# State rows in one transfer per half, and the division of a on VectorE: an attention and two MoE layers on one core

## The reference, cut to what matters

```
B, H, S, Ns, D = 8, 8, 512, 32, 64
scores = scale * x @ state^T          # [B, H, S, Ns]
a  = exp(scores - max);  a  /= a.sum(-1)  + 1e-9       # "a": rows over the states
xread = a @ state
scores2 = scale * state @ x^T         # the same products, transposed
a2 = exp(scores2 - max); a2 /= a2.sum(-1) + 1e-9
sread = a2 @ x
x = concat([xread, sread], rows)      # 8 batches of 512 + 32 rows, 512 columns
x = ((x @ w1) * (x @ w2)) @ w3 @ w_out            # moe1, d_ff 1024
h = x @ w_in;  out = (h - tanh(h)) @ w_out2       # moe2, d_ff 2048
```

## Time and profile before

| | |
|---|---|
| time, median of 3 runs | 1258.31 us (1258.15 to 1258.31) |
| the profiled execution's own time | 1258.3 us |
| its span | 1256.2 us |
| busy: TensorE, VectorE, ScalarE, GpSimd | 1245.0, 792.2, 546.5, 16.0 us |
| granted clock of TensorE | 1.00 up to 1254 us |
| front stage | 0 to about 112 us; ys to 121, moe1 to about 513 us |
| transfers | 63.75 MB, nearly all in the first 66 us at above 400 GB/s |

### The profile page before, as it was taken

How to read it: one execution, slowest core, us unless ns; L and a number is a source line. 1 busy time by engine, 2 the same in 40 slices (tenths; PEclk the granted TensorE clock), 3 DMA queues, 4 the chain that set the end, 5 groups by cost and what they waited for, 6 DMA issues and landing times. The chain is left out here.

```text
span 1256.2 us, 17133 instructions
## 1 busy us (share of the span) xinstructions
PE 1245.0 (99%) x6652; PEld 1003.6 (80%) x6652; DVE 792.2 (63%) x1282; ACT 546.5 (44%) x1023; POOL 16.0 (1%) x14
## 2 busy tenths in 40 slices
PE   8999999999999999999999999999999999999998
PEld 6779777777777778888888888888888888888887
DVE  4656555545454434788667676676676676776766
ACT  5663333333333333545444344344444444444443
POOL 0000000000000000000000000000000000000000
PEclk9999999999999999999999999999999999999999
DMA  9930100000000112211100101001001001010000
GB/s 373 401 115 27 59 34 1 34 35 1 34 34 1 52 53 81 84 51 51 51 10 14 44 18 51 1 17 50 0 17 50 8 9 50 17 42 0 8 34 17
DMA packets 18109, 63.75 MB, mean 51 GB/s; under 512 B 1920, under 2 KB 3200, under 8 KB 14080
## 3 DMA queue, kind: packets, MB, share of 16 engines
q1 hardware_dynamic: 17712, 62.59, 13.6%
q10 hardware_dynamic: 336, 0.33, 0.1%
HBM read 45.09 MB, written 17.83 MB: 50 GB/s over the span
## 5 line engine op out<-in xcount | busy, mean ns | idle before, releaser
L1208 ACT ACTIVATE hq<-bank 128x512 f32<-128x512 f32 (+1 forms) x144 | 82.8, 575 | 395.7 <-PE bank L1334 395.7
L1279 DVE TENSOR_TENSOR hw<-hw,hq 128x512 f32<-128x512 f32 (+1 forms) x144 | 95.5, 663 | 194.9 <-ACT hw L1219 194.7
L1334 PE MATMUL bank<-ysp_hi,wi_hi 128*128 128x512 f32 (+1 forms) x576 | 217.3, 377 | 0.0
L1334 PE MATMUL bank<-ysp_lo,wi_hi 128*128 128x512 f32 (+1 forms) x576 | 217.3, 377 | 0.0
L1334 PE MATMUL bank<-ysp_hi,wi_lo 128*128 128x512 f32 (+1 forms) x576 | 217.3, 377 | 0.0
L1360 PE MATMUL wide<-wz_hi,gsp_hi 128*128 128x512 f32 x544 | 212.5, 391 | 1.4 <-DVE gsp_lo L1269 1.3
L1360 PE MATMUL wide<-wz_lo,gsp_hi 128*128 128x512 f32 x544 | 211.8, 389 | 0.0
L1360 PE MATMUL wide<-wz_hi,gsp_lo 128*128 128x512 f32 x544 | 211.8, 389 | 0.0
L1334 PEld LDWEIGHTS bank<-ysp_hi,wi_hi 128*128 128x128 f32 x576 | 108.4, 188 | 20.6
L1334 PEld LDWEIGHTS bank<-ysp_lo,wi_hi 128*128 128x128 f32 x576 | 108.2, 188 | 20.4
L1334 PEld LDWEIGHTS bank<-ysp_hi,wi_lo 128*128 128x128 f32 x576 | 108.3, 188 | 20.0
(11 more groups left out here) (127 smaller groups left out, 1748.5 us busy)
## 6 DMA issues: line engine op xcount, KB each, us to landing
y_dram<-ysb SPq DMA_DIRECT2D x8, 1024.0 KB, 4.3
out<-ysb SPq DMA_DIRECT2D x8, 1024.0 KB, 4.6
yr<-y_dram SPq DMA_DIRECT2D x28, 256.0 KB, 4.1
xs<-in_x_rows SPq DMA_DIRECT2D x6, 1024.0 KB, 9.0
xT<-in_x_cols SPq DMA_DIRECT2D x5, 1024.0 KB, 10.6
w_raw<-in_moe_w SPq DMA_DIRECT2D x8, 512.0 KB, 8.3
wi_raw<-in_moe_w_in SPq DMA_DIRECT2D x4, 1024.0 KB, 7.1
raw<-in_moe_w_out SPq DMA_DIRECT2D x16, 256.0 KB, 2.6
```

The lines of the kernel that those rows point to most:

```text
L1208: act.activation(hq[:, f % 2, 0:w], ph[f % 2][:, 0:w], ACT.Square).then_inc(sq_done, 1)
L1279: dve.tensor_tensor(u, u, q, ALU.mult).then_inc(w2_done, 1)
L1334: mm = pe.matmul(ph[f % 2][:, 0:w], wi[s][c][:, f * P:(f + 1) * P], ysp[k][u][c][:, 0:w], start=c + m == 0, stop=c == KC - 1 and m == LAST)
```

## The change

Four edits:

- The state rows of a half are stored by one transfer (four batches) in place of four.
- The division of `a` by its sums is done by VectorE, directly before the transpose back, in place of GpSimd. In the front stage batch 0's division and transpose back stand behind `split_w3(6)`.
- In the rounds of the front stage VectorE does `split_sr` and `split_w3` ahead of batch 0's sum and reciprocal (e = 4) and of its division and transpose (e = 5).
- SyncE issues the load of w3's slice 2 ahead of x by columns of batch 2, and slice 5 and x of batch 5 ahead of x of batch 6.

```diff
-    def gpsimd_scale(self, pool, e):
-        pool.wait_ge(self.row_inv, e + 1)
+    def vector_scale(self, dve, e):
+        dve.wait_ge(self.row_inv, e + 1)
         a = self.room(e)
-        pool.tensor_tensor(a, a, self.rinv[:, :].unsqueeze(2).to_broadcast([P, J * H, NS]), ALU.mult).then_inc(self.scaled, 1)
+        dve.tensor_tensor(a, a, self.rinv[:, :].unsqueeze(2).to_broadcast([P, J * H, NS]), ALU.mult).then_inc(self.scaled, 1)
...
         for e in range(2, 5):
+            if e == 2:
+                load_w3(sp, e)
             load_xT(sp, e)
-            load_w3(sp, e)
+            if e > 2:
+                load_w3(sp, e)
             for n in ((0,), (1, 2), (3,))[e - 2]:
                 load_w(sp, n)
             load_xs(sp, e)
-        load_xT(sp, 6)
         load_w3(sp, 5)
         load_xT(sp, 5)
+        load_xT(sp, 6)
...
-        for e in range(B):
-            rows.gpsimd_scale(pool, e)
...
+            split_sr(e - 1)
+            if e < NF1 - 1:
+                split_w3(e + 1)
             if e == 4:
                 rows.vector_sum(dve, 0)
                 rows.vector_invert(dve, 0)
             if e == 5:
+                rows.vector_scale(dve, 0)
                 rows.vector_back(dve, 0)
-            split_sr(e - 1)
-            if e < NF1 - 1:
-                split_w3(e + 1)
             empty_prod(e)
...
         rows.vector_invert(dve, 1)
+        rows.vector_scale(dve, 1)
         rows.vector_back(dve, 1)
...
                     if f == 7:
+                        rows.vector_scale(dve, b + 2)
                         rows.vector_back(dve, b + 2)
...
     def store_states(eng, j):
-        for n in range(P // NS):
-            eng.dma_start(out_v[j * (P // NS) + n, S:ROWS, :], ob[n * NS:(n + 1) * NS, j, :]).then_inc(o_out, 16)
+        batches = slice(j * (P // NS), (j + 1) * (P // NS))
+        eng.dma_start(out_v[batches, S:ROWS, :], ob[:, j, :]).then_inc(o_out, 16)
...
-        sp.wait_ge(o_out, 16 * 2 * B)
+        sp.wait_ge(o_out, 16 * (B + 2))
```

## The result

The changed kernel takes 1263.25 us (median of six runs, 1263.21 to 1265.79) against 1258.41 us for the kernel before on the same chip (six runs, 1258.15 to 1258.56): a ratio of 1.0042 (that of the medians is 1.0038), 95% interval 1.003 to 1.0054. By the medians it is slower by 4.8 us, where 4.3 had been forecast. The sixth took 1265.79.

What follows compares the result with a forecast made beforehand. The prediction took TensorE, busy 1245.0 of 1256.2 us, to bound the kernel, followed by a tail of stores. 1258.3 + 0.2 (front) + 4.1 (tail) = 1262.6 us; range 1260.0 to 1265.0.

Steps and rivals of the forecast that it cites:

- Tail: Final state-row stores: each merged transfer uses the same four DMA engines, 64 rows each at 0.10 us; +4.1 us.
- 16 engines: Rival for the final stores: all 16 engines take each merged transfer; −0.6 us there, 1257.9 us in all; chance 0.13.
- different engines for the two halves: Rival for the final stores: four engines each, but not the same four; +1.6 us, 1260.1 in all; chance 0.06.
- The fixed 1.56: Final stores: the fixed us per transfer, 1.8 − 2 × 0.12, to which the time of the rows is added.
- the shorter issues: Final stores: SyncE's and ScalarE's issue, 0.4 in place of 1.8 us, gains nothing because the engines end last.
- The landings of 5 to 9 us: Sign in the changed profile's final stores: transfers landing that late would show the forecast right, near 2.5 us wrong.
- Front: Front stage: gains at batches 2 and 5 against a loss at batch 6, −0.25 − 0.75 + 1.2 = +0.2 us.
- Iteration 5: Front stage, batch 5: the 1.26 us wait for w3's low part goes, exponentials come later; gain 0.65 to 0.8 us.
- Iteration 6: Front stage, batch 6: division and transpose back on VectorE delay tokens_max(6) and the exponentials; loss 1.1 to 1.3 us.
- The loads at batch 2: Front stage: w3 lands some 2.5 us sooner, x at about 28.0; gain 0.20, up to 0.28 us.
- The exchange of x 5 and x 6: Front-stage loads: brings x 5 forward; no wait for either is in the trace, so it gives nothing.
- The other seven divisions: ys and moe1 stages: moving them to VectorE costs nothing; if cover is gone, 0.1 us twice.

Runs made afterwards that it cites:

- store_only: The kernel before with only the merged stores, one transfer per half: 1263.29 us, ratio 1.0037.
- store_pairs: The kernel before with two batches per store transfer, two transfers per half: 1268.77 us, ratio 1.0084.
- store_serial: The kernel before with merged stores, ScalarE issuing its half only when SyncE's has landed: 1266.59 us, ratio 1.0064.
- front_x6_back: The changed kernel with stores in four transfers per half and x of batch 6 loaded ahead again: 1258.40 us, ratio 1.0003.
- low_ahead_w3: The kernel before with w3's low part ahead of batch 0's sum and w3's slice 2 loaded ahead of x of batch 2; division on GpSimd: 1257.77 us.
- front_only: The changed kernel with the stores in four transfers per half as before: 1258.57 us, ratio 1.0001.
- gap_division: front_x6_back with batch 0's division and transpose back at the head of round 5, where VectorE is idle: 1257.27 us, ratio 0.999.

## Why the forecast came out right, point by point

**Tail, +4.1 forecast, +4.8 measured.** The mechanism held: four engines, the same for both halves, 64 rows each, 256 packets of 2 KB and 8 small ones, a share near 0.25, 9.1 us from the first issue to the end. The rivals of 16 engines and of different engines for the two halves fall by the share of 0.26 in the changed kernel, and again by `store_only` and `store_pairs`. But that +4.1 is so near +4.8 is in part luck: two errors offset each other. A row costs 2048 B / (102 / 4 GB/s) = 0.080 us, the lower bound, and not the 0.10 that I took; 64 rows are 5.1 and not 6.4 us, −1.3. Against that stands a term that I didn't have: 1.56 + 5.1 + 0.4 makes 7.1, and it was 9.1, so the slow begin costs 2.0 us. In `store_serial` the same sum for one half gives 1.95 (6.07 − 1.56 − 32 × 0.080). The fixed 1.56, worked out from transfers on 16 engines, was thus the mis-sized term: for these it is about 3.5 (1.56 + 1.95 to 2.0). The remark on the shorter issues (nothing gained) was right. That the chain would end in a transfer was wrong: it ends in VectorE's `ysb`, as before, since it doesn't follow the last stores. The landings of 5 to 9 us can't be read, as the profile gives none for these transfers.

**Front, +0.2 forecast, between 0.0 and +0.1 measured** (+4.84 us for the change and +4.77 for the stores alone, +0.05 for the rest, each against the kernel before on its chip). Its steps:

*Iteration 5.* As forecast: the wait of 1.26 goes, a wait of 0.33 for the exponentials takes its place (0.4 expected), `tokens_max(5)` at 58.46 (58.57 expected). The gain is 0.9 us from 62.31 to 61.41, of which 0.06 was there already at the transposes of batch 4 (52.16 against 52.22); 0.75 had been expected.

*Iteration 6.* The division costs 1.17 us in `front_x6_back`, within 1.1 to 1.3. In the changed kernel it lies under the wait for x, so the TensorE wait of 1.2 us foretold for its trace is not there; there VectorE's `tokens_max(6)` comes at 68.78 and waits 0.34.

*The loads at batch 2.* x landed 8.4 us after its issue at 19.58, at 28.0 as forecast, and w3's slice 6.3 us after 19.20, at 25.5. The scores of batch 2 start at 29.33 without a wait on a transfer, and the 0.20 is gone from the trace. ScalarE's wait for the slice, 0.53 in the earlier trace rows, is gone as well. But the forecast took for fixed a wait of TensorE that varies: four of seven traces with the old order lack it (see `low_ahead_w3`), so its absence here does not credit the exchange, and the times show too little to tell the gain from nothing. One figure ahead of the prediction is off: of the 63.75 MB some 25 MB, not nearly all, move in the first 66 us (343 GB/s up to 18 us, 399 from there to 66).

*The exchange of x 5 and x 6 "gives nothing".* This is the step that failed. I looked only for a wait that the exchange could remove, and didn't ask what the queue has to do while the load now in front waits for its buffer. From 46 to 50 us it moves 217 GB/s in the changed kernel's trace, where it moved 402, and 315 in the next two, where it moved 420; the rows of x for batch 5 land 9.8 us after their issue (8.0 before), and TensorE waits 1.60 us for them. The sum survived it because that wait and the division's stall cover each other: in the traces the changed kernel loses 1.72 us there and `front_x6_back` 1.17, not the sum of two losses. The 0.55 between them is as much as this execution lies above its kernel's median, so in a usual execution the exchange may cost nothing at all; in the medians it stays unresolved. What a long wait can cost besides is in the trace of `front_only`, with the fall of the granted clock.

*The other seven divisions.* Nothing, as forecast: TensorE's wait for `pm` in moe1 is 0.4 us before and after. The `pm` of the earlier trace rows comes 5.52 us after its forerunner in place of 5.43, the 0.1 us foretold, and it is covered.

**What was left on the table.** `gap_division` takes 1257.27 us, 1.25 us less than the kernel before on its chip (1258.52) and 6.0 less than the changed one: the same edits of VectorE's work, with the division ahead of `split_sr` and `split_w3` in place of behind them, x 6 left ahead and the stores left in four pieces.

**Open.** Why a merged transfer begins slowly, and why one of ScalarE's issues takes 2.0 us beside it. The traces show only that the begin has nearly the same total rate with four engines (12 to 29 GB/s) and with two (29), so it does not go with the number of engines at work. Not run: a merged transfer with the 32 rows outermost in place of the four batches. It would tell whether the loss comes from the merging or from the order of the dimensions, and whether the slow begin goes with it.

## What to carry to other kernels

Before merging stores, look at the outermost dimension, here that of the destination: four transfers of 32 rows used all 16 DMA engines, one of [4, 32, 512] uses four and costs 4.8 us more at the end of a kernel. Work given to a busy engine is priced by its place in the round: look for idle time in front of the instruction that will follow it, not at the engine's share. When a load is moved, ask what the queue does while the load now ahead waits for its buffer, and when a wait disappears, ask which later ones it had covered.

## What the hardware showed that was not expected

- A 256 KB store cut over four engines begins at 12 to 29 GB/s for about two microseconds, then runs at 102 GB/s. With two 128 KB stores per half, cut over two engines, it was 29 for five microseconds and then 51. Alone, the 256 KB store takes 6.1 us, where a 256 KB load over 16 engines lands in 2.6.
- Beside such a transfer an issue from another engine took 2.0 us in place of 0.46 (one profiled execution).
- GpSimd's division beside VectorE: the subtraction with two operands in SBUF took 2.82 in place of 1.23 us, the maximum over 128 x 1024 stayed at 1.21, and a bias of 128 x 2 took 0.32 in place of 0.17.
- After a wait of 2.12 us TensorE's granted clock fell to 0.50 for some three microseconds (one execution); after one of 1.60 us it stayed at 1.00.
